# The last group of an MLP makes its outputs in tiles of 384 tokens, feature by feature

## The reference

```
h = relu(x @ w_in)              # w_in 512 x 2048
x = (h * h) @ w_out             # w_out 2048 x 512
for e in range(4):              # the experts, w1 512 x 1024, w2 1024 x 512
    out += p[:, e] * (relu(x @ w1[e]) @ w2[e])
```

## Time and profile before

| | |
|---|---|
| runs, us | 613.37, 612.75, 612.43; median 612.75 |
| profiled execution, us | 612.54 |
| its span, us | 610.7 |
| granted TensorE clock | 1.00 |
| PE busy (a matmul in flight) | 602.6 us, 99% |
| DVE, ACT, POOL busy | 60%, 36%, 46% |

### The profile page before, as it was taken

One profiled execution on the slowest core, in us unless ns is written; L12 is line 12 of the kernel. 1 busy time (PEld: TensorE's weight loads), 2 busy tenths in 40 slices (PEclk: granted clock), 3 DMA queues, 4 the chain that ended last, 5 costly groups with the idle time before them and its releaser, 6 DMA issues.

```text
span 610.7 us, 11302 instructions
## 1 busy us (share of the span) xinstructions
PE 602.6 (99%) x4347; PEld 561.8 (92%) x4347; DVE 366.5 (60%) x797; ACT 221.7 (36%) x508; POOL 279.3 (46%) x230
## 2 busy tenths in 40 slices
PE   7899999999999999999999999999999999999998
PEld 6789999999999999998988989989989989989987
DVE  6787595746847878735636536636536446446452
ACT  2688373514524645511511421422332322232210
POOL 4679844551560587961560451462443353350300
PEclk9999999999999999999999999999999999999999
DMA  7953020220110220120220110220120030010012
GB/s 254 288 171 139 1 70 2 70 70 2 69 70 2 70 70 0 71 70 1 70 69 1 70 69 1 70 71 0 65 75 1 25 114 1 7 64 1 1 52 104
DMA packets 16677, 36.92 MB, mean 60 GB/s; under 512 B 2032, under 2 KB 2800, under 8 KB 16624
## 3 DMA queue, kind: packets, MB, share of 16 engines
q1 hardware_dynamic: 16544, 36.05, 17.3%
q10 hardware_dynamic: 80, 0.15, 0.1%
HBM read 33.84 MB, written 2.36 MB: 59 GB/s over the span
## 4 chain that ended last, share of the span: by engine, by line
PE 94%; DMA 3%; SPq 1%; DVE 1%; issue 0%; POOL 0%; ACT 0%; ACTq 0%
PE ps L1374 31%; PE ps L1376 31%; PE ps L1375 31%; DMA k_buf<-in_k 3%; PE ps L1364 1%; PE ps L1321 0%; DVE k_buf L1127 0%; PE ps L1334 0%; SPq L419 0%; SPq L412 0%; POOL prob L621 0%; SPq L438 0%; DVE ssum L919 0%; ACT y L705 0%; DVE t_form L944 0%
## 5 line engine op out<-in xcount | busy, mean ns | idle before, releaser
L1374 PE MATMUL ps<-xf_hi,wa_hi 128*128 128x288 f32 x672 | 199.3, 297 | 0.0
L1375 PE MATMUL ps<-xf_lo,wa_hi 128*128 128x288 f32 x672 | 198.3, 295 | 0.0
L1376 PE MATMUL ps<-xf_hi,wa_lo 128*128 128x288 f32 x672 | 197.6, 294 | 0.0
L574 POOL TENSOR_TENSOR wb_lo<-raw_b,wb_hi 128x512 fp32r<-128x512 f32 x48 | 61.0, 1307 | 175.9 <-ACT wb_hi L726 175.9
L1374 PEld LDWEIGHTS ps<-xf_hi,wa_hi 128*128 128x128 f32 x672 | 126.0, 187 | 0.9 <-ACT wa_hi L717 0.2
L1375 PEld LDWEIGHTS ps<-xf_lo,wa_hi 128*128 128x128 f32 x672 | 126.1, 188 | 0.5
L1376 PEld LDWEIGHTS ps<-xf_hi,wa_lo 128*128 128x128 f32 x672 | 126.5, 188 | 0.0
L1376 PE MATMUL ps<-wb_hi,h_lo 128*128 128x512 f32 (+1 forms) x292 | 113.0, 387 | 0.0
L1375 PE MATMUL ps<-wb_lo,h_hi 128*128 128x512 f32 (+1 forms) x292 | 113.0, 387 | 0.0
L1374 PE MATMUL ps<-wb_hi,h_hi 128*128 128x512 f32 (+1 forms) x292 | 112.8, 386 | 0.0
L1118 DVE SCALAR_TENSOR_TENSOR y<-ps,p_norm,y 128x512 f32<-128x512 f32 (+1 forms) x64 | 47.5, 742 | 102.3 <-PE ps L1376 102.3
(11 more groups left out here) (88 smaller groups left out, 759.7 us busy)
## 6 DMA issues: line engine op xcount, KB each, us to landing
raw_a<-in_wa SPq DMA_DIRECT2D x48, 256.0 KB, 3.5
raw_b<-in_wb SPq DMA_DIRECT2D x24, 512.0 KB, 4.0
q_buf<-in_q SPq DMA_DIRECT2D x8, 288.0 KB, 4.4
k_buf<-in_k SPq DMA_DIRECT2D x15, 144.0 KB, 3.9
v_loc<-in_v_near SPq DMA_DIRECT2D x4, 512.0 KB, 4.3
result<-y SPq DMA_DIRECT2D x8, 256.0 KB, 2.0
v_str<-in_v_far SPq DMA_DIRECT2D x4, 384.0 KB, 4.4
v_loc<-in_v_last SPq DMA_DIRECT2D x4, 64.0 KB, 5.3
```

The lines of the kernel that those rows point to most:

```text
L574: nc.gpsimd.tensor_tensor(wb_lo[:, :, cols], raw_b[:, :, cols], wb_hi[:, :, cols].bitcast(F32), ALU.subtract).then_inc(s_wb_lo, 1)
L1374: nc.tensor.matmul(dst, a_hi, b_hi, start=first, stop=False)
L1375: nc.tensor.matmul(dst, a_hi, b_lo, start=False, stop=False)
L1376: return nc.tensor.matmul(dst, a_lo, b_hi, start=False, stop=last)
```

## The change

B6 and B7 become wide too: B6 makes the tokens 0 to 767 in 8 tiles and B7 the tokens 768 to 1151 in 4, of 384 tokens each. In these two, the order stays feature by feature (in B6 both thirds of a feature tile one after the other). The counts that the forms wait for follow, through half_done and y_count. DVE's program changes in B7: set 3's T1 stands behind tile 1, and set 3's pieces T2, T3 and T4 of the first feature tile all stand behind the last tile, ahead of the T2 piece of the second. PE's wait for the next A stage's C21 now comes ahead of the first tile that reads it, which is B6's second tile.

```diff
         def wide(t):
-            return 2 <= t < BLOCKS1 - 2
+            return 2 <= t < BLOCKS1
+
+        def last_group(t):
+            return BLOCKS1 - 2 <= t < BLOCKS1
+
+        def half_done(t, kt):
+            return (kt + 1) * y_count(t) // 2
...
             if wide(t):
-                third, dt = divmod(i, KT)
+                if last_group(t):
+                    dt, third = divmod(i, y_count(t) // KT)
+                else:
+                    third, dt = divmod(i, KT)
                 third += 2 * (t % 2)
...
# x_high, on ACT
-                    act.wait_ge(s_y, y_tiles(BLOCKS1 - 4 + i) + (KT if k == B11 else 2 * KT))
+                    act.wait_ge(s_y, y_tiles(BLOCKS1 - 4 + i) + half_done(BLOCKS1 - 4 + i, 0 if k == B11 else 1))
...
# t_forms, on DVE
-                        dve.wait_ge(s_y, y_tiles(BLOCKS1 - 4 + i) + KT)
+                        dve.wait_ge(s_y, y_tiles(BLOCKS1 - 4 + i) + half_done(BLOCKS1 - 4 + i, 0))
...
# half_form, on DVE
-                dve.wait_ge(s_y, y_tiles(BLOCKS1 - 4 + i) + KT + 2 * (kt + 1))
+                dve.wait_ge(s_y, y_tiles(BLOCKS1 - 4 + i) + (kt + 3) * y_count(BLOCKS1 - 4 + i) // KT)
...
# DVE's program, in the loop over the tiles of a B stage
-                        if t >= BLOCKS1 - 2 and i == KT - 1:
+                        if last_group(t) and i == half_done(t, 0) - 1:
                             t_forms(t - BLOCKS1 + 4, T1)
 
-                        if t >= BLOCKS1 - 2 and i > KT:
-                            half_form(t - BLOCKS1 + 4, (T2, T3, T4)[i - KT - 1], 0)
+                        if t == BLOCKS1 - 2 and i > KT:
+                            half_form(2, (T2, T3, T4)[i - KT - 1], 0)
                         if t == BLOCKS1 - 1 and i < 3:
                             half_form(2, (T2, T3, T4)[i], 1)
                     if t == BLOCKS1 - 1:
+                        for k in (T2, T3, T4):
+                            half_form(3, k, 0)
                         half_form(3, T2, 1)
...
# PE, outputs_of_block
-                    if wide(t) and c == 0 and i == KT:
+                    if wide(t) and part == 1 and dt == 0:
 
                         pe.wait_ge(s_h_lo, tile_count(t + 1, C21, 1))
```

## The result

| | before | after |
|---|---|---|
| runs, us | median 612.36 (610.84 to 613.37, 8 runs) | median 616.69 (614.05 to 617.14, 8 runs) |
| profiled execution / its span, us | 612.54 / 610.7 | 617.07 / 615.3 |
| mean granted clock of the profiled execution | 1.00 | 0.997 |

The ratio after/before is 1.0065, 95% interval 1.0051 to 1.0079: slower by 3.1 to 4.8 us.

What follows compares the result with a forecast made beforehand. TensorE's matmul stream was taken as the bound (in flight 602.6 of 610.7 us). Saving -0.48 plus stall 2.86 gave +2.4 us: 612.54 became 614.9, plus 0.21 for the median, 615.1; range 612.1 to 616.0.

Steps and rivals of the forecast that it cites:

- What the tiles save: B6 and B7: 144 matmuls of 384 columns replace 192 of 288, at measured spacings; saves 0.48 us.
- The moved wait for h: B6's second output needs A7's C21 h_lo, done at 207.80, due at 208.78; margin 1.0 us, cost nothing.
- DVE's additions: B6 and B7: 12 additions of 384 replace 16 of 288; 5.8 us in all, about as much as before.
- set 2: First half's forms for A8: POOL's low parts begin at 230.86 instead of 225.35; margin over 1 us, cost nothing.
- The four forms behind the last output: After B7: four DVE pieces each wait for a POOL instruction, delaying A8's c_block; PE stalls 2.9 us ahead of M7.
- Behind the stall: After A8's M7: third sums keep 0.2 us margin, B8 in time; bound 0 to 0.4 us, taken as nothing.
- The first rival: After B7: first DVE piece gets ahead of POOL, three POOL instructions met; stall 1.5 to 1.8 us; chance 0.17.
- The second: After B7: the four pieces run at 0.45 us each, no stall, only the 0.48 saving left, 612.3 us; chance 0.13.
- The third rival: A8 after the idle: clock falls to 1.2 GHz, four products take double, 6.4 us more, up to 621.5; chance 0.08.

Runs made afterwards that it cites:

- The hold on POOL: Changed kernel with POOL waiting ahead of set 2's T3 until DVE has made five pieces of set 3; median 613.00 us, ratio 1.0015.
- the filled kernel: Changed kernel with 19 matmuls of 288 columns put into PE's idle between A8's M6 and M7; median 614.76 us, ratio 1.0036.
- tiles of 288: Changed kernel with B6 and B7 back at 288-token tiles, DVE's new order kept; median 612.87 us, ratio 1.0010.
- early pieces: Changed kernel with set 3's three first-tile pieces moved behind B7's third addition, POOL's T2 of set 2 waiting for them; 612.55 us, ratio 1.0009.

## Why the prediction was right and wrong

**What the tiles save:** 0.48 worked out, 0.49 measured. The measured spacing of B4 held for B6 and B7.

**The moved wait for h, DVE's additions, set 2:** right. The last h_lo of C21 is done at 207.88 + 0.45 = 208.33, due at 209.32. POOL's series starts 231.39 - 207.24 = 24.15 us after B6; worked out were 230.86 - 206.70 = 24.16.

**The four forms behind the last output:** right to some hundredths. With B6 0.54 later than assumed, the pieces had to end at 234.54, 236.14, 237.74 and 239.37; they end at 234.53, 236.15, 237.75 and 239.32. The stall is 2.86 us, as forecast. The hold on POOL shows that the cause is the one named.

**Behind the stall:** right, no other wait; without the clock the stretch would be 47.36 + 2.86 = 50.22, and the filled kernel has 50.32.

**The first rival** (the first piece gets through) did not come: 0.10 us were worked out between POOL's start and DVE's, 0.10 were there, and POOL had it. That was close: with tiles of 288, a piece issued 0.08 ahead of POOL's start got through. **The second** (no stall) fell too.

**The third rival is the step that failed.** "The stall costs more than itself" had a chance of 0.08, and the forecast and the range were made without it. It was the rule: in nine of twelve runs the mean clock was 0.997, and both traces of such runs have the fall behind the idle. Its size was wrong the other way, 6.4 us as a bound against 1.5 measured, because I let all four remaining products run at 1.2 GHz, where some 3.3 us did, from 241.0 to 244.3. With this term and the 0.1 of wider spacings the sum is -0.49 + 2.86 + 1.60 = +3.97, and 612.36 + 3.97 = 616.3, beside the measured 616.69. Without it the forecast was 615.1, and the range ended at 616.0. The forecast also stood on 612.75, the median of three runs; on the 612.36 of eight it would have been 614.7, and the three executions of the changed kernel at clock 1.000 have a mean of 614.5. So the rest of the sum was right, and the range was missed by the clock's term alone. I gave it little weight since no row showed such a fall. But no row showed a PE idle of that length either, so the trace was no evidence against it. The prediction should have given this rival a far larger chance. The Trainium skill ("TensorE: Matmul & The Clock Gate", section "Part 1: The HAM clock gate") says that activity releases the throttle and that without it the clock is at half; the runs here agree, with 1.00 ahead of the idle and 0.50 from 1.2 us behind it on, for 3.3 us of full work.

The direction, slower by more than 0.2%, was forecast with 0.67 and came.

## What to carry to other kernels

A saving on a full TensorE shortens the time that the other engines have for what lies behind it: ask which queue loses its cover, and lay it out instruction by instruction (here that came out to 0.05 us) before counting the saving. A DVE instruction with both inputs in SBUF that came while POOL was at work on low parts ended 0.31 us behind the POOL instruction that it met, and each further one in a row cost a whole POOL instruction. So keep such pieces from standing between a result of TensorE and the sum that it waits for. To put them ahead of POOL's series, or to hold POOL, removed the stall here, but POOL's delay or the next meeting of the two took the 0.48 us back. And an idle of TensorE that is longer than any that the trace has in the full stretches may have a price of its own behind it: give the clock's fall a term and a fair chance in the sum.

## What was not expected of the hardware

- The clock fell not in the idle but after its end, 1.2 us behind it in one trace and 0.3 in the other, and for 3.3 to 3.4 us in both. With the one idle of 2.86 us the mean clock was 0.997 in nine of twelve runs; in three it was 1.000, and no trace was taken of these. One idle of 1.40 us (ten runs; all lengths here as in the list of waits, which has the 2.86 as 2.69) or two of 1.12 and 1.14 (eight runs) never brought the mean clock under 0.999, and neither did any of the 68 runs of the kernel before. The kernels with early pieces and with tiles of 288 had one run each at 0.997 (615.71 and 615.81 us, about 3 us over their medians), though their traces, taken of other runs, have no such idle in these stages. The cause of these two is open, so an idle as in the changed kernel is not shown to be the only thing that brings the clock down.
- Where POOL's series runs on, DVE pieces in a row alternate with its instructions one by one (four and four in the changed kernel). A POOL instruction that follows such a piece is recorded 0.2 us longer (1.65 against 1.44).
- From B8's first matmul to the last one's start all eleven profiled executions take 353.27 to 353.34 us: what is won or lost ahead passes through to the end undiminished. B6's start differs more between executions (204.88 to 208.45 us from the span's start) than any of these edits saves, and that is why the runs can hardly tell such savings from nothing.
